# A new first phase: channel MLP in blocks of 512 tokens, scores and values as 64x64 pieces in four quarters of the array, queries turned by VectorE, straight code

## The reference, cut to what matters

```python
# 1. attention inside chunks of 64 tokens, 8 heads of 64
scores = (1 / sqrt(64)) * q_c @ k_c.T            # 64 x 64 for each chunk and head
attn = exp(scores - max); attn /= sum(attn) + 1e-9
x = attn @ v_c                                   # -> x[batch, 576, 512]
# 2. mixer: tokens, then channels
u = x + (relu(x.T @ w_tok1) @ w_tok2).T          # 576 -> 256 -> 576 tokens
x2 = u + relu(u @ w_ch1) @ w_ch2                 # 512 -> 1536 -> 512 channels
# 3. gated unit over tokens
h = relu(x2 @ w_in); a, g = halves of h
g = layernorm(g);  g = w_spatial @ g + b_spatial
out = (a * g) @ w_out
```

## Time and profile before

| | |
|---|---|
| time, median of 3 runs (lowest to highest) | 1360.36 us (1359.75 to 1360.47) |
| profiled execution, its own time | 1359.22 us |
| its span, first to last instruction | 1357.4 us |
| PE busy | 1343.2 us, 99% |
| DVE / ACT / POOL busy | 528.3 / 418.6 / 64.2 us |
| prologue, up to the first `up` | 45.7 us |
| one loop body (batch), from 325.0 to 440.4 | 115.4 us |
| phase 2, from 937.8 | 419.6 us |

### The profile page before, as it was taken

The page is one execution under the profiler, slowest core; times in us unless marked ns, Lnnn a source line. Parts: engine busy times, 40 slices in busy tenths (PEclk is TensorE's granted clock), DMA queues, the critical chain, the costliest instruction groups (busy, mean ns, idle before and its releaser), DMA issues.

```text
span 1357.4 us, 26091 instructions
## 1 busy us (share of the span) xinstructions
PE 1343.2 (99%) x9485; PEld 1291.7 (95%) x9485; DVE 528.3 (39%) x1167; ACT 418.6 (31%) x843; POOL 64.2 (5%) x45
## 2 busy tenths in 40 slices
PE   9999999999999999999999999999999999999998
PEld 9999999999999999999999999999998998998997
DVE  3343234234224324423432342234563463463461
ACT  6532133123213312321321331123433433433332
POOL 3800000000000000000000000122000000000000
PEclk9999999999999999999999999999999999999999
DMA  9523021212302211220230210312021021021002
GB/s 251 127 53 67 21 42 42 40 38 40 66 22 44 54 26 43 55 45 25 53 67 21 42 34 1 130 47 90 1 87 55 0 76 63 0 70 70 1 1 70
DMA packets 183429, 70.57 MB, mean 52 GB/s; under 512 B 159184, under 2 KB 171088, under 8 KB 183312
## 3 DMA queue, kind: packets, MB, share of 16 engines
q1 hardware_dynamic: 183312, 68.98, 20.2%
HBM read 50.05 MB, written 18.87 MB: 51 GB/s over the span
## 4 chain that ended last, share of the span: by engine, by line
PE 99%; issue 1%; ACT 0%; POOL 0%; POOLq 0%
PE bank L1053 31%; PE bank L1206 23%; PE bank L1188 23%; PE bank L1131 5%; PE bank L1115 5%; PE bank L1071 4%; PE bank L1144 3%; PE bank L1106 1%; PE bank L1079 1%; PE bank L1122 1%; PE bank L1225 1%; PE bank L1149 0%; PE bank L1148 0%; PE bank L1082 0%; PE bank L1165 0%
## 5 line engine op out<-in xcount | busy, mean ns | idle before, releaser
L832 DVE SCALAR_TENSOR_TENSOR hidl<-bank,hidh 128x256 fp32r<-128x256 f32 (+1 forms) x192 | 88.0, 458 | 438.6 <-ACT hidh L649 438.6
L1206 PE MATMUL bank<-hidh,w2h 128*128 128x256 f32 (+1 forms) x768 | 237.1, 309 | 0.0
L1188 PE MATMUL bank<-uh,w1h 128*128 128x256 f32 (+1 forms) x768 | 228.3, 297 | 7.8 <-issue 7.8
L1188 PE MATMUL bank<-uh,w1l 128*128 128x256 f32 (+1 forms) x768 | 227.3, 296 | 0.0
L1188 PE MATMUL bank<-ul,w1h 128*128 128x256 f32 (+1 forms) x768 | 227.3, 296 | 0.0
L1206 PE MATMUL bank<-hidh,w2l 128*128 128x256 f32 (+1 forms) x768 | 227.1, 296 | 0.0
L1206 PE MATMUL bank<-hidl,w2h 128*128 128x256 f32 (+1 forms) x768 | 226.7, 295 | 0.0
L649 ACT ACTIVATE hidh<-bank 128x256 fp32r<-128x256 f32 (+1 forms) x192 | 78.9, 411 | 456.6 <-PE bank L1188 456.6
L1188 PEld LDWEIGHTS bank<-uh,w1h 128*128 128x128 f32 x768 | 145.8, 190 | 9.9 <-issue 9.3
L1206 PEld LDWEIGHTS bank<-hidh,w2h 128*128 128x128 f32 x768 | 145.4, 189 | 1.6
L1206 PEld LDWEIGHTS bank<-hidl,w2h 128*128 128x128 f32 x768 | 145.6, 190 | 0.5
(11 more groups left out here) (158 smaller groups left out, 2356.7 us busy)
## 6 DMA issues: line engine op xcount, KB each, us to landing
x2l_raw<-x_scratch SPq DMA_DIRECT2D x32, 256.0 KB, 4.3
out<-out_tile SPq DMA_DIRECT2D x32, 256.0 KB, 2.0
qn<-in_q SPq DMA_DIRECT2D x30, 256.0 KB, 3.2
vn<-in_v SPq DMA_DIRECT2D x30, 256.0 KB, 3.9
kn<-in_k SPq DMA_DIRECT2D x448, 16.0 KB, 1.7
x_scratch<-x_half SPq DMA_DIRECT2D x8, 640.0 KB, 4.2
x_scratch<-x_half SPq DMA_DIRECT2D x8, 512.0 KB, 3.3
w1l_raw<-in_moe_w_ch SPq DMA_DIRECT2D x6, 512.0 KB, 9.1
```

The lines of the kernel that those rows point to most:

```text
L832: return nc.vector.scalar_tensor_tensor(lo, src, 0.0, hi.bitcast(F32), op0=ALU.max, op1=ALU.subtract)
L1188: last = nc.tensor.matmul(hid_bank[g % 2][:, 0:width(h)], w, x, start=(c == 0 and e == 0), stop=(c == KC - 1 and e == 2))
L1206: last = nc.tensor.matmul(acc_bank[c][:, 0:n], w, x, start=(f == 0 and e == 0), stop=(f == KF - 1 and e == len(ops) - 1))
```

## The change

Phase 1 is written anew; phase 2 computes the same by the same instructions.

- **Blocks.** The 4608 tokens are taken as 9 blocks of 512, whatever the batch. Block j holds the rest of batch j-1 (64 j tokens) and the first 512 - 64 j tokens of batch j. Each of 12 `up` and 12 `down` has 12 matmuls of 512 columns. Token mixing of a batch is given out in two parts, `UA` (into block b) and `UB` (the remaining 64 + 64 b tokens, into block b+1), in place of `U0` and `U1`.
- **Scores and values.** Each 64x64 product is a matmul of its own, with a 64x64 stationary operand in one of four quarters of the array, chosen by the partitions of the operands (head of the pair) and of the output (chunk): 16 for a tile in `SC` and 16 in `PV` in place of 8 and 8. The two heads of a pair go to two banks. The zeros in `q_t` and `p_t`, and the two half copies on ACT that made them, are gone.
- **Queries** come by 32x32 blocks as keys do and are turned by DVE; `TQ` and `TK` are left in the prologue alone. Values come by 4 transfers for each tile (2 for the fifth).
- **Straight code** in place of all loops, in both phases. Side jobs and loads follow new tables (`PLAN`, `REST`; SP's order below). `q_t` and `k_t` have one buffer after the prologue, `hidh` and `hidl` two in place of three.
- The low part of the residual is added by POOL (`add_low`) in place of DVE. In the prologue, normalisation goes from POOL to DVE.
- The first loads of batch 1 stand between the loads of the channel weights, and ACT splits four of six groups of these weights in block 0 in place of two.

```diff
-    SIDE = {0: [("U1", 0), ("U1", 1)], 1: [("U1", 2), ("U1", 3)], 2: [("TQ", 0)], 3: [("SC", 0)], 4: [("TQ", 1)],
...
+    GROUPS = [("up", 0), ("up", 1)]
+    for f in range(KF):
+        GROUPS += [("down", f)] + ([("up", f + 2)] if f + 2 < KF else [])
+    PLAN = {2: "SC.0", 5: "SC.1", 6: "PT.0", 7: "PV.0", 8: "SC.2", 9: "PT.1", 10: "PV.1", 11: "SC.3", 12: "PT.2",
+            13: "PV.2", 14: "SC.4", 15: "PT.3", 16: "PV.3", 17: "PT.4", 18: "PV.4", 19: "M.0", 20: "M.1",
+            21: "UA.0 UA.1", 22: "UA.2 UA.3"}
+    REST = {3: "UB.0 UB.1", 4: "UB.2 UB.3"}
...
+            def load_blocks(buf, src, b, t, loaded):
+                for h2 in range(2):
+                    for e in range(D // BLK):
...
+                        for g in range(PAIRS):
...
+                            sp.dma_start(dst[:, g, :, :],
+                                         part.rearrange("(j r) e -> r j e", r=BLK)).then_inc(loaded[t], DMA)
+            def load_qk(b, t):
+                n = later(b, t)
+                if n >= 2:
+                    sp.wait_ge(q_t_ready, NT + n - 1)
+                    sp.wait_ge(k_t_ready, NT + n - 1)
+                load_blocks(qn, q_in, b, t, q_loaded)
+                load_blocks(kn, k_in, b, t, k_loaded)
...
+                if g == 1:
+                    load_qk(1, 0)
+                if g == 2:
+                    load_v_next(1, 0)
+                    load_qk(1, 1)
+                if g == 3:
+                    load_v_next(1, 1)
+            load_qk(1, 2)
...
+            for j in range(B - 1):
+                b = j + 1
+                if j > 0:
+                    store_x2(j - 1)
+                more = b + 1 < B
+                load_qk(b, 3)
+                load_qk(b, 4)
+                load_v_next(b, 2)
+                if more:
+                    load_qk(b + 1, 0)
+                load_v_next(b, 3)
+                if more:
+                    load_qk(b + 1, 1)
+                load_v_next(b, 4)
+                if more:
+                    load_qk(b + 1, 2)
+                    load_v_next(b + 1, 0)
+                    load_v_next(b + 1, 1)
...
+            def turn(b, t):
...
+                dve.wait_ge(side_full, number[("SC",) + before])
+                for buf, dst, loaded, ready in ((qn, q_t, q_loaded, q_t_ready), (kn, k_t, k_loaded, k_t_ready)):
+                    dve.wait_ge(loaded[t], loads)
+                    nc.vector.transpose(dst[:, :, 0:rows(t)].bitcast(U32),
+                                        blocks(buf, b, t).bitcast(U32).rearrange("p (g s) -> p g s", g=PAIRS)
+                                        ).then_inc(ready, 1)
...
                 elif kind == "SC":
...
                     for g in range(PAIRS):
-                        for a in range(2 if t < KS else 1):
-                            c0 = (2 * g + a) * CHUNK
-                            last = nc.tensor.matmul(bank[:, c0:c0 + CHUNK], q_t[:, t % 2, g, a, :],
-                                                    k_t[:, t % 2, g, a * CHUNK:(a + 1) * CHUNK], start=True, stop=True)
+                        for e in range(2):
+                            for a in range(n // CHUNK):
+                                r, s = slice(e * D, (e + 1) * D), slice(a * CHUNK, (a + 1) * CHUNK)
+                                last = nc.tensor.matmul(two[s, e, g * CHUNK:(g + 1) * CHUNK], qt[r, g, s], kt[r, g, s],
+                                                        start=True, stop=True)
...
+            for j in range(NB):
+                for g, (kind, f) in enumerate(GROUPS):
+                    if kind == "up":
+                        up(j, f)
+                    else:
+                        down(j, f)
+                    for job in behind(j, g):
+                        side_job(job)
```

More of the change, by code:

```diff
@@ L16, with jobs @@
 BLK = 32
[L19 to L28, removed]
+def jobs(b, text):
+    return [(kind, b, int(t)) for kind, t in (x.split(".") for x in text.split())]
 def build(nc, q, k, v, w_tok1, w_tok2, w_ch1, w_ch2, w_in, w_spatial, b_spatial, w_out, out, x2_dram):
@@ L91, in build, with share @@
[L91 to L97, removed]
+    def share(kind, b):
+        cut = BW - REM * b
+        return (0, cut, b, REM * b) if kind == "UA" else (cut, S, b + 1, 0)
@@ L518, in store_out @@
                                      out_tile[bb * REM:(bb + 1) * REM, n % 2, :]).then_inc(s, DMA)
-            def pair(j, last):
-                if not last:
+            for j in range(NP):
+                if j < NP - 1:
                     sp.wait_ge(full, j * NJ + job_no(("U", NU - 1)))
@@ L764, in pair @@
                         o_out(j, m)
-                    if not last and X2_AT <= n < X2_AT + X2_PIECES:
+                    if j < NP - 1 and X2_AT <= n < X2_AT + X2_PIECES:
                         split_x2(j + 1, n - X2_AT)
-            for piece in range(X2_PIECES):
-                split_x2(0, piece)
-            act.wait_ge(x2_ready, 1 + 2 * B)
-            with act.Fori(0, B // 2 - 1) as j:
-                pair(j, False)
-            pair(B // 2 - 1, True)
         @block.vector
         def _(dve):
-            dve.sem_inc(acc_free, KC)
@@ new lines, in _ @@
+            for j in range(NB):
+                if j > 0:
+                    residual(j - 1)
+                for g, (kind, f) in enumerate(GROUPS):
+                    if kind == "up":
+                        hidden(j, f)
+                    if j == 0 and g == 1:
+                        turn(1, 0)
+                    for job in behind(j, g - 1) if g > 0 else []:
+                        if job[0] == "SC":
+                            softmax_norm(job[1], job[2])
+                    for job in behind(j, g):
+                        if job[0] == "SC":
+                            softmax_shift(job[1], job[2])
+                            n = later(job[1], job[2]) + 1
+                            if n < (B - 1) * NT:
+                                turn(1 + n // NT, n % NT)
+                        elif job[0] in TWO_PART:
+                            side_job(job)
@@ L937, in stats @@
+            for piece in range(KC):
+                split_x2(0, piece)
+            residual(NB - 1)
+            for b in range(4, 8):
+                dve.sem_inc(free[b], 1)
+            for piece in range(KC, X2_PIECES):
+                split_x2(0, piece)
             def stats(j, n):
```

898 lines of the change are left out of this document (422 added, 476 removed), and 6 rows, old and new, of the table SIDE.

## The result

| | before | after |
|---|---|---|
| time, median of 4 runs (lowest to highest) | 1360.15 us (1359.75 to 1360.47) | 1415.37 us (1415.09 to 1416.30) |
| ratio, with 95% interval | | 1.0407 [1.0389, 1.0425] |
| span of the profiled execution | 1357.4 us | 1413.8 us |
| prologue, up to the first `up` | 45.7 us | 55.1 us |
| blocks 0; 1 to 5; 6; 7; 8 | | 136.6; 111.8 to 114.8; 93.9; 77.7; 65.2 us |

The change makes the kernel 4.1% slower, where 2.0% (1387 us) was forecast. The time lies inside the range of 1285 to 1425. The direction and the mechanism were right, but the loss of 55 us is twice the forecast one of 27.

The account below looks back on a forecast made before the run. SP's issuing was to set the pace: PE alone 1282 us, plus 69 for blocks 1 to 6 and 35 for block 0, is 1386, with 1.1 for the median 1387 us; range 1285 to 1425.

Parts of the forecast that it names:

- cycle: From one SC.0 to the next, SP's 138 issues delay PV.4: 108.3 us a block, 11.5 more than PE needs.
- An issue at 0.494 us: On SP's queue each load issue takes 0.494 us, the lowest earlier value; 138 issues take 68.2 us.
- rival E: On SP's queue an issue takes 0.527 us: 32 us more, 1419 us; no separate chance, included in SP-pace's 0.47.
- Rival D: After PE's gaps the clock drops, about 2 us each, seven times: 14 us, 1401; no separate chance, within SP-pace's 0.47.
- Six cycles: In blocks 1 to 6, PE waits ahead of PV.4 for SP's issues: 69 us lost in all.
- Block 0: Tile 2 loads are issued near 80 us, so PV.4 starts at 150 instead of 115: loss 35 us.
- Point 5: SC and PV on PE as small matmuls in array quarters: cost 93.5 us instead of 132.0, gain 38.5.
- The middle case: In SC and PV, neighbouring quarters overlap in twos, 0.0305 us a record: gain 38.5 us.
- best case: In SC and PV, quarters overlap four ways without any other limit: cost 58 us.
- Points 1, 2, 3 and 7: On PE: 512-wide blocks gain 26.2 us, no loop ends 7.8, no TQ in seven batches 16; UA and UB lose 9.
- point 7: On PE, narrow parts of UA and UB in six batches cost extra, 0 to 18.5 us; 9 taken.
- Rival A: PE stays the bound because SP's issues take under 0.41 us: faster, 1283 us, chance 0.20.

Follow-up runs that it names:

- experiment 4: The changed kernel with unneeded matmuls filling PE's gaps ahead of PV.3 and PV.4: 1418.11 us; filling only the last gap, ahead of PV.4: 1406.74 us.
- experiment 6: The changed kernel with query loads on POOL's queue: 1292.87 us; last kernel, also with POOL's loads reordered, batch 0 values on POOL and prologue jobs reordered: 1275.30 us.
- experiment 5: The changed kernel with queries loaded whole and turned by TensorE again: 1388.34 us; second kernel, with x2 stores first and TQ in other banks: 1304.30 us.
- experiment 3's first kernel: The changed kernel with every 64x64 matmul of SC and PV issued twice: 1435.35 us, ratio 1.0561.

## Why the prediction was right or wrong

The forecast of 1387 us rested on a cycle (SC.0, 138 issues, landing, PV.4, next SC.0) and on PE's side. The cycle is there as described, in blocks 1 to 5. Its terms:

| term of the cycle | forecast | measured, block 4 |
|---|---|---|
| SC.0 to the first issue | 2.9 | 2.8 |
| 138 issues | 68.2 (0.494 each) | 71.3 (0.517) |
| landing, signals | 2 | 2.1 |
| PV.4 to the end of the next SC.0 | 35.2 | 36.6 |
| sum | 108.3 | 112.8 |

1. **An issue at 0.494 us.** Mis-sized. 0.494 was the lowest of the earlier trace rows; the 16s of block 4 run from 7.45 to 8.75 us, and values (64 KB pieces) take 0.65 each, where 0.494 was taken for them too. That is 3.1 us a block. The truth lies between the forecast and rival E (0.527).
2. **Rival D, the clock.** It came true beside the forecast. Priced as an alternative, it should have been a term of the sum, since 11.5 us of idleness were forecast and the row that shows the cost was at hand. It is in the last term of the table. With the last gap filled (experiment 4) that term is 34.0 in the same block, so the clock costs 2.6 us there, where 2 was priced, and PE's other work was 1.2 shorter than forecast. The Trainium skill ("TensorE: Matmul & The Clock Gate", Part 1) says that a long idle stretch brings the clock down, and the trace agrees at 7.9 us. Issues (3.1) and clock (2.6), less PE's shorter work (1.2), make up the 4.5 us of the cycle, 24 us in five blocks with the 114.8 of the first.
3. **Six cycles.** The forecast counted blocks 1 to 6. The wait for the values of batch 6 lies in block 5, and block 6 loads nothing for a batch after it: 93.9 us, not 108.3. So 14 us were forecast too many, and it is luck that this error hides a third of the others.
4. **Block 0.** It ended at 191.7 us, where the forecast had 45.7 + 132 = 177.7: 14 us more. PV.4 started at 160 against 150. The loads of tile 2 were issued from 70.8 to 86.7, 7 later than forecast (query and key issues at 0.51 us, value issues at 0.65, and of the 5 us that were to be saved on waiting for the queues only 2 were), and the 138 issues behind them took 71.6 us. The 4 us left lie behind PV.4, where the lower clock stands again.
5. **The prologue.** It is 9.4 us longer than before, and the forecast took it as unchanged. But in the changed kernel this is no loss of its own: the chain that ended last runs through SP's issues from 1.9 us to PV.4 of block 0, so by it a shorter prologue would only have made PE wait longer there. The length counts in the kernels where PE is the bound, and there the last kernel of experiment 6 gave 4.7 back: SC and PV, once they fill both banks of a pair, wait for each other. The chain from 0 to 165 us:

```profile
by line: SPq L459 62.9%; SPq L449 14.2%; issue 8.0%; SPq L441 3.9%; SPq L492 3.0%; PE hid L1147 2.2%; SPq L490 1.8%; DMA vn<-in_v 1.5%; PE side L1105 0.7%; SPq L486 0.7%; SPq L483 0.4%; SPq L487 0.4%; SPq L467 0.1%
```

6. **Point 5, SC and PV.** The middle case was taken (twos, 0.0305 a record, a cost of 93.5 us and a gain of 38.5) and is wrong. 80 visits at 0.83 us are 66 where 132.0 stood, a gain of 66. That is near the prediction's best case, four ways without any other limit: a cost of 58, a gain of 74. The Trainium skill ("TensorE: Matmul & The Clock Gate", Part 3) has matmuls in different tiles of the array run together. Here the trace agrees: a quarter gets 8 of the 32 records, 8 x 0.061 = 0.49, and 32 x 0.061 = 1.95 us of work fit into the 0.63 of the visit only if all four quarters work at once in some of it. The visit of the fifth tile (0.61) says the same. The least distance of some 25 ns that the prediction quotes from the Trainium skill ("TensorE: Matmul & The Clock Gate", Part 1) does not hold here: 32 records start within 0.63 us, 0.020 each.
7. **Points 1, 2, 3 and 7.** 512-wide steps are 0.227 as forecast, and no wait stands at a block's end. TQ was priced at 2.3 us a batch, and experiment 5 shows about 3. UA and UB: 64, 128 and 192 columns all step by 0.11 in the products, so 6 batches of narrow parts cost 7 us (24 matmuls in each, worked out from the steps of both widths), 9 was taken. In point 7 itself the extra for 64 columns should read 67 ns, not 57 (97 less 64 x 0.47), which moves its bound of 18.5 by 0.5.

PE alone was forecast at 97 us a block and takes 92.0 to 93.9; the 3.5 us of point 5 are most of it. Rival A's total of 1283 is met by the kernel without query loads (1282.35) only because its longer prologue (57.1 us), its block 0 (102.4) and the last two blocks fill what point 5 had missed.

The ledger, in spans, from 1384 (the 1386 of the sum less the 1.8 between time and span) to the measured 1413.8: up to the end of block 0 +14, blocks 1 to 5 +24, block 6 -14, blocks 7 and 8 +6 (142.9 us, where the forecast's total leaves 137 for them). What was missed in the last two was not taken apart. So the failed steps are sizes (the issue at 0.494 us in place of 0.517; block 0), one omission (the clock, priced at 2 us a gap as rival D but left out of the sum, measured 2.6) and one count (block 6). The chance of 0.20 for rival A and its bound (an issue under 0.41 us) were sound: in no run did sixteen issues of the loads take less than 7.35 us, 0.46 each.

The kernel's design was right on PE and lost on SP. With the same blocks, quarters and turns, and its query loads on a second queue, it is 5.0% faster than before.

## What to carry to other kernels

Before work is moved from a busy engine to transfers, follow the issuing queue from the release of a buffer to the user of the last transfer behind it, and multiply the issues by the 0.5 us that this study measured. A sum over a loop body misses it, twice in this study. Then look at what else is in the same stretch: moving values ahead of loads that nobody waits for yet gave 64 us, a second queue 122. Behind a gap of 7 to 8 us on the path add the 1.6 to 2.6 us that the lower clock cost here.

## What was not expected of the hardware

- Four 64x64 quarters of the array work at once, and the step inside one of them stays near the 0.061 us of the earlier trace rows: 32 records over four quarters take 0.63 us, 16 over two take 0.61. Twice as many records in the same quarters took 1.24 us (548.98 to 550.22 in experiment 3's first kernel).
- Narrow fp32r products have a floor. With `t2h` and `t2l`, 128 columns take 0.11 us to the next start, as 64 and 192 do, where a quarter of the 0.227 of 512 would be 0.057. The turns of x against `ident_r`, also 128 columns, step by 0.08. PE's timeline of the changed kernel:

```profile
748.80 0.28 PE L1048 MATMUL side<-t2h,ml 128*128 128x128 f32 x1
748.91 0.25 PE L1055 MATMUL side<-ident_r,xh 128*128 128x128 f32 x1
```

```profile
260.31 0.77 PE L1108 MATMUL side<-vn,p_t 64*64 64x64 f32 x32 [2.06 <-DMA vn<-in_v]
```

- SP is hardly slowed by POOL's issuing: sixteen of its loads take 7.4 to 9.4 us beside POOL's and 7.4 to 9.2 without. What POOL's pace would be alone no run shows.
